# Late weight tiles and attention tiles at multiples of 64 bytes, and a start signal sent ahead of the first loads

## The chip, the cores and the metric

One Trainium2 chip, one NeuronCore of it. The metric is the device time of one execution in microseconds (us); lower is better. The engines are TensorE (PE; its weight loads are PEld), VectorE (DVE), ScalarE (ACT), GpSimd (POOL) and SyncE (SP), which issues most transfers.

## The reference

```python
# attention: q, k, v of (2, 8, 768, 64); proj of (64, 6)
q_bits = einsum('bhsd,dk->bhsk', q, proj) > 0          # 6 hash bits a row, the same for k
mask = q_bucket[:, :, :, None] == k_bucket[:, :, None, :]
scores = where(mask, q @ k.T / 8, -1e9)
attn = exp(scores - max); attn /= sum(attn) + 1e-9
x = (attn @ v).transpose(0, 2, 1, 3).reshape(1536, 512)
# layer 0: w_in (512, 2048), w_out (2048, 512)
h = x @ w_in
g = (a0 + a1*h + a2*h*h + a3*h**3) / (1 + |b0|*|h| + |b1|*h*h + 1e-6)
x = g @ w_out
# layer 1: the same sizes
h = x @ w_in
x = (h - tanh(h)) @ w_out
```

All of it is float32.

## The kernel before, in words

**Attention.** The 16 heads are worked in 8 pairs of two. A pair has 12 tiles of 128 queries by 768 keys. For each tile TensorE computes the scores (4 matmuls of 384 columns, L249), turns the tile before it with six transposes against `ident` (L375, from `E` into `turn_ps`) and, in 3 of 4 positions of a schedule, multiplies by v (4 matmuls of 384 columns, L333 and L335). VectorE takes the row minimum (L567), ScalarE the exponential (L455); the turned tile is split into a rounded part and a rest (`pt_hi` by ScalarE, `pt_lo` by VectorE). The operands of the scores are `qA`, `kA`, `qB`, `kB`, two sets of them for the two heads.

**The two layers.** All products are three matmuls of 512 columns, of rounded parts and rests (`_hi`, `_lo`). The 1536 tokens are 3 chunks of 512; the hidden 2048 are 16 tiles. That makes 48 tiles in each layer, 96 in all, numbered t. For tile t `pe_g1` makes h from x with 12 matmuls (L789, stationary operand `win`), and `pe_g2` multiplies g by `wout` with 12 matmuls (L818). In layer 0 `wout` is the stationary operand, in layer 1 it is the one that moves. TensorE's order is fixed: `pe_g1(t + 4)`, `pe_g2(t)`, `pe_g1(t + 5)`, and so on; the first four `pe_g1` stand between the last pieces of the attention. In layer 0 VectorE has seven operations of 512 columns for each tile; in the first chunk it also splits most weights, one `win_lo` and one `wout_lo` for a tile, since the weights of each layer are split when they are first used. `pe_g2(t)` waits for `g_lo(t)` of VectorE.

**Where tiles lie.** SBUF tiles are given out one behind the other. Each begins at a multiple of 32 bytes. The activations `x_hi`, `x_lo`, `g_hi`, `g_lo`, the early weights (`win0` to `win3`, `wout0`, `wout1`) begin at byte 16512 or a whole number of 128 bytes behind it. Behind the early weights stand five small tiles of 4 to 16 bytes, 32 bytes each. Their 160 bytes are two and a half times 64. So everything behind them begins at 32 bytes past a multiple of 64: the late weights (`win4` to `win15`, `wout2` to `wout15`, hi and lo), and the attention's `v_nat`, `bits`, `qA` to `kB` and `pats`. Then `counts`, 8 bytes in 32, brings `proj_bd`, `ident`, `E`, `v_hl`, `pt_hi` and `pt_lo` to a multiple of 64 (64 bytes past a multiple of 128); behind the small `row_` tiles `x_raw`, `x_pair`, `x_norm` and `scale` are at 32 past again. The late weights take the same space as the attention's tiles, once these are free.

**The start.** `pe_scores` of the first tile of a head waits for 128 counts of `ops0` or `ops1` for each pair done. From the second pair on these come from the eight copies of 16 counts that fill the operands. The first pair's operands are written by the engines themselves, so SyncE adds the 128 counts by hand (L1216, L1217). It does so behind all its starting loads, the six early weights among them.

Of the kernel before, what the change touches and what calls it, by code (L numbers as in the profile page):

```python
# [6 lines left out]
F32 = mybir.dt.float32  # L7
# [6 lines left out]
P = 128  # L14
# [16 lines left out]
def build(nc, q, k, v, proj, w_in1, w_out1, coef_a, coef_b, w_in2, w_out2,  # L31
          identity, patterns, bit_counts, out):
    B, H, S, D = q.shape
# [25 lines left out]
    top = ExitStack()  # L59
    att = ExitStack()  # L60
    mlp = ExitStack()
    sb = lambda ctx, name, shape, dt: ctx.enter_context(nc.sbuf_tensor(name, shape, dt))
# [11 lines left out]
            for names in ADDED_BY.values() for name in names}  # L74
    loads = {name: top.enter_context(nc.semaphore("s_" + name))
             for name in ["ident", "consts", "coefs", "ready", "coef", "proj", "q", "k", "v", "out", "ops0", "ops1",
                          "scale_out0", "scale_out1", "scale_in0", "scale_in1", "shift0", "shift1", "pool_here", "sync_here"]
             + ["t_turn", "t_q", "t_k", "t_dots", "t_bits", "t_hot", "t_hot_q", "t_hot_k",
                "t_hi_q", "t_hi_k", "t_hi_kb", "t_lo", "t_op1"]
             + [f"w_in{j}" for j in range(J)] + [f"w_out{j}" for j in range(J)]}  # L80
# [10 lines left out]
    with top:  # L91
# [37 lines left out]
        q_one = sb(top, "q_one", [P, 1], F32)  # L129
        sum_eps = sb(top, "sum_eps", [P, 1], F32)  # L130


        v_nat = sb(att, "v_nat", [P, 2, T * D], F32)
        bits = sb(att, "bits", [P, HALF], BF16)
# [1 line left out]
               for e in range(2)]  # L136
        opA, opB = [ops[e][0] for e in range(2)], [ops[e][1] for e in range(2)]
        pats = sb(att, "pats", [P, 4, P], BF16)
        counts = sb(att, "counts", [P, 2], F32)
        proj_bd = sb(att, "proj_bd", [P, 2, KB], F32)  # L140
        ident = sb(att, "ident", [P, P], F32)
        E = sb(att, "E", [P, RING, S], F32)
        v_hl = [sb(att, f"v_hl{e}", [P, T, 2, D], F32R) for e in range(2)]
        pt_hi = sb(att, "pt_hi", [P, 2, T, HALF], F32R)
        pt_lo = sb(att, "pt_lo", [P, 2, T, HALF], F32R)
        row_min = sb(att, "row_min", [P, RING], F32)
        row_sum = sb(att, "row_sum", [P, 2, T], F32)
        row_eps = sb(att, "row_eps", [P, 2, T], F32)
        row_inv = sb(att, "row_inv", [P, 2, T], F32)
        x_raw = [sb(att, f"x_raw{e}", [P, S], F32) for e in range(2)]  # L150
        x_pair = sb(att, "x_pair", [P, S], F32)
        x_norm = sb(att, "x_norm", [P, S], F32)
        scale = sb(att, "scale", [P, S], F32)
        slot = [ps(att, f"slot{i}", [P, 2, 512]) for i in range(2)]
        turn_ps = [ps(att, f"turn_ps{i}", [P, 512]) for i in range(2)]
        pv_ps = ps(att, "pv_ps", [P, 512])
# [332 lines left out]
        def dve_sum(eng, c):  # L489
            eng.wait_ge(mlp_sems["low"], c + 1)  # L490
            mine, _, cols = own_and_other(c)
            eng.tensor_tensor(x_raw[0][mine, cols], pv_ps[mine, 0:HALF], x_raw[0][mine, cols],
                              ALU.add).then_inc(mlp_sems["sum"], 1)
# [275 lines left out]
        def pe_g1(eng, t):  # L769
            layer, c, j = place(t)  # L770
            _, w_hi, w_lo = w_in_slot[j]
            if c == 0:
                if layer == 0 and j < POOL_IN:
                    eng.wait_ge(mlp_sems["early_lo"], POOL_TILES.index(("in", j)) + 1)
                else:
                    eng.wait_ge(mlp_sems["w_in_lo"], split_in_count(layer, j))
            if layer == 0 and c == 1 and j == 0:
                eng.wait_ge(sems["xlo"], BIAS + PAIRS - 1)
                eng.wait_ge(mlp_sems["last_lo"], 1)
            if layer == 1 and j == 0:  # L780
                eng.wait_ge(mlp_sems["x2_lo"], 4 * (c + 1))
            if t >= TILES_LAYER + 4:
                eng.wait_ge(mlp_sems["g"], t - 3)
            elif t >= 4:
                eng.wait_ge(mlp_sems["h_free"], t - 3)
            for kt in range(KT):
                ws = slice(kt * P, (kt + 1) * P)
                for n, (w, x) in enumerate(((w_lo, x_hi), (w_hi, x_hi), (w_hi, x_lo))):
                    mm = eng.matmul(h_ps[t % 4][:, :], w[:, ws], columns(x, kt, c),  # L789
                                    start=kt + n == 0, stop=kt == KT - 1 and n == 2)  # L790
            mm.then_inc(mlp_sems["h"], 1)

        def pe_g2(eng, t):
            layer, c, j = place(t)
            _, w_hi, w_lo = w_out_slot[j]
            hi, lo = g_hi[:, t % TEMPS, :], g_lo[:, t % TEMPS, :]
            if c == 0:
                if layer == 0 and j < POOL_OUT:
                    eng.wait_ge(mlp_sems["early_lo"], POOL_TILES.index(("out", j)) + 1)
                else:  # L800
                    eng.wait_ge(mlp_sems["w_out_lo"], split_out_count(layer, j))
            eng.wait_ge(mlp_sems["g_lo"], t + 1)
            if t == 0:
                eng.wait_ge(sems["pt_lo"], BIAS + 2 * TILES * PAIRS)
                eng.wait_ge(mlp_sems["sum"], GROUPS)
            for i in range(4):
                cs = slice(i * P, (i + 1) * P)
                if j == 0 and t > 0:
                    if layer == 0 or c == 0:
                        eng.wait_ge(mlp_sems["x2_raw"], 4 * (t // J - 1) + i + 1)  # L810
                    else:
                        eng.wait_ge(mlp_sems["y"], 4 * (c - 1) + i + 1)
                if layer == 0:
                    terms = ((w_lo[:, cs], hi), (w_hi[:, cs], hi), (w_hi[:, cs], lo))
                else:
                    terms = ((hi[:, cs], w_lo[:, :]), (hi[:, cs], w_hi[:, :]), (lo[:, cs], w_hi[:, :]))
                for n, (l, r) in enumerate(terms):
                    mm = eng.matmul(acc[i][:, :], l, r if layer else r[:, :], start=j + n == 0,  # L818
                                    stop=j == J - 1 and n == 2)
                if j == J - 1 and i < 3:  # L820
                    mm.then_inc(mlp_sems["acc"], 1)
            mm.then_inc(mlp_sems["g2"], 1)
# [253 lines left out]
        with nc.Block() as block:  # L1076

            @block.sync
            def _(eng):
# [86 lines left out]
                def load_weight(layer, kind, j):  # L1166
                    if kind == "in":
                        if layer == 1:
                            eng.wait_ge(mlp_sems["h"], 2 * J + j + 1)
                        w = (w_in1, w_in2)[layer]  # L1170
                        eng.dma_start(w_in_slot[j][0][:, :].rearrange("r (k n) -> r k n", n=P),  # L1171
                                      w.rearrange("(k r) n -> r k n", r=P)[:, :, j * P:(j + 1) * P]
                                      ).then_inc(loads[f"w_in{j}"], 16)
                    else:
                        if layer == 1:
                            eng.wait_ge(mlp_sems["g2"], 2 * J + j + 1)
                        w = (w_out1, w_out2)[layer]
                        eng.dma_start(w_out_slot[j][0][:, :], w[j * P:(j + 1) * P, :]
                                      ).then_inc(loads[f"w_out{j}"], 16)

                def sync_att(p, turn=True):
                    if turn:
                        load_qk(p + 2, 0)
                        load_qk(p + 2, 1)
                    copy_split(p + 1, 0)
                    if not is_zero(p):
                        shift(p - 1, 1)
                    scale_out(p, 0)
                    copy_hot(p + 1, 0)
                    load_v(p + 1)  # L1190
                    copy_split(p + 1, 1)
                    copy_hot(p + 1, 1)
                    scale_in(p, 0)
                    shift(p, 0)
                    scale_out(p, 1)
                    scale_in(p, 1)

                for e in range(2):
                    eng.dma_start(nat[0][:, :, e, :], q_d[0, :, e]).then_inc(loads["q"], 16)
                eng.wait_ge(loads["ready"], 1)  # L1200
                for x in range(2):
                    for e in range(2):
# [10 lines left out]
                    load_weight(0, "in", j)  # L1213
                for j in range(EARLY_OUT):
                    load_weight(0, "out", j)

                eng.sem_inc(loads["ops0"], 128)  # L1217
                eng.sem_inc(loads["ops1"], 128)
                sync_att(0)
                with eng.Fori(1, PAIRS - 2) as p:  # L1220
                    sync_att(p)
# [131 lines left out]
```

## Time and profile before

| | us |
|---|---|
| median of 3 runs | 783.09 (781.21 to 783.39) |
| the profiled execution | 782.13 |
| its span | 780.0 |
| TensorE busy | 766.5 (98%) |
| VectorE busy | 537.1 (69%) |
| ScalarE busy | 478.8 (61%) |
| GpSimd busy | 155.7 (20%) |

The span runs from the first to the last instruction that the profiler recorded; 2.13 us of the execution lie around it. In the timeline a row gives the start and the length of an instruction. The length of a matmul contains its latency: consecutive ones overlap, so TensorE's pace is read from the distance between starts.

### The profile page before, as it was taken

How to read it: one execution, taken by the hardware profiler on the slowest of the kernel's cores; microseconds unless marked ns; L12 is line 12 of the kernel's file. 1: busy time of each engine (PE TensorE's matmuls, PEld its weight loads, DVE VectorE, ACT ScalarE, POOL GpSimd, SP SyncE). 2: the span in 40 equal slices, each digit the busy share in tenths (PEclk: the TensorE clock that was granted, in tenths of full speed). 3: DMA queues.
4: the chain of work that ended last, by engine and by line, in shares of the span. 5: the costliest groups of instructions: out<-in, count | busy, mean ns of one | idle time of the engine just before them, and what ended most of it. 6: DMA issues, size and time to landing. Idle time of an engine off the chain costs nothing.

```text
span 780.0 us, 11965 instructions
## 1 busy us (share of the span) xinstructions
PE 766.5 (98%) x3840; PEld 645.0 (83%) x3840; DVE 537.1 (69%) x856; ACT 478.8 (61%) x940; POOL 155.7 (20%) x133
## 2 busy tenths in 40 slices
PE   4999999999999999999999999999999999999998
PEld 3899999999998877888888888888888888888886
DVE  3888988988997999999888888946442322232222
ACT  4888988988997878787666867755432222212221
POOL 5774575566566000000000000000000000000000
PEclk8999999999999999999999999999999999999999
DMA  7579778777744320000000232320000100001001
GB/s 192 122 171 208 171 174 190 184 177 175 170 116 122 119 82 1 1 0 1 1 0 15 56 106 84 106 67 1 1 0 1 55 0 1 1 14 41 0 1 55
DMA packets 65243, 58.11 MB, mean 75 GB/s; under 512 B 31792, under 2 KB 50480, under 8 KB 65200
## 3 DMA queue, kind: packets, MB, share of 16 engines
q1 hardware_dynamic: 63488, 57.09, 29.1%
q10 hardware_dynamic: 1712, 0.46, 0.3%
q8 instruction: 25, 0.41, 0.2%
q14 instruction: 18, 0.15, 0.1%
HBM read 29.57 MB, written 3.19 MB: 42 GB/s over the span
## 4 chain that ended last, share of the span: by engine, by line
PE 97%; DMA 1%; issue 1%; SPq 1%; ACT 0%; ACTq 0%; DVE 0%
PE acc L818 34%; PE h_ps L789 34%; PE slot L249 9%; PE turn_ps L375 8%; PE pv_ps L333 4%; PE pv_ps L335 4%; PE aux_ps L262 1%; PE aux_ps L271 1%; PE aux_ps L282 1%; DMA k_nat<-in_k 1%; SPq L1171 0%; PE turn_ps L292 0%; ACT E L455 0%; SPq L1091 0%; ACT kA L427 0%
## 5 line engine op out<-in xcount | busy, mean ns | idle before, releaser
L789 PE MATMUL h_ps<-x_hi,win_hi 128*128 128x512 f32 x384 | 152.1, 396 | 0.0
L789 PE MATMUL h_ps<-x_hi,win_lo 128*128 128x512 f32 x384 | 151.4, 394 | 0.0
L789 PE MATMUL h_ps<-x_lo,win_hi 128*128 128x512 f32 x384 | 150.9, 393 | 0.0
L839 ACT ACTIVATE g_hi<-pol 128x512 fp32r<-128x512 f32 x96 | 60.9, 634 | 128.2 <-PE acc L818 105.5
L1008 DVE TENSOR_TENSOR g_lo<-pol,g_hi 128x512 fp32r<-128x512 f32 x96 | 65.9, 686 | 102.1 <-ACT g_hi L839 101.9
L609 DVE TENSOR_TENSOR pt_lo<-turn_ps,pt_hi 128x384 fp32r<-128x384 f32 x192 | 97.9, 551 | 18.9 <-ACT pt_hi L516 17.2
L516 ACT ACTIVATE pt_hi<-turn_ps 128x384 fp32r<-128x384 f32 x192 | 84.2, 494 | 16.4 <-PE turn_ps L375 14.7
L567 DVE TENSOR_REDUCE row_min<-slot 128x1 f32<-128x768 f32 x96 | 90.5, 943 | 4.1 <-PE slot L249 4.1
L455 ACT ACTIVATE E<-slot,row_min 128x768 f32<-128x768 f32 x96 | 88.0, 917 | 5.4 <-DVE row_min L567 2.7
L789 PEld LDWEIGHTS h_ps<-x_hi,win_lo 128*128 128x128 f32 x384 | 72.1, 188 | 17.6
L789 PEld LDWEIGHTS h_ps<-x_lo,win_hi 128*128 128x128 f32 x384 | 72.1, 188 | 16.9
L789 PEld LDWEIGHTS h_ps<-x_hi,win_hi 128*128 128x128 f32 x384 | 72.1, 188 | 16.7
L1002 DVE TENSOR_TENSOR pol<-h_ps,mag 128x512 f32<-128x512 f32 x48 | 33.2, 691 | 70.7 <-ACT mag L862 70.7
L375 PE MATMUL turn_ps<-ident,E 128*128 128x128 f32 x576 | 80.2, 275 | 0.0
L862 ACT ACTIVATE mag<-h_ps 128x512 f32<-128x512 f32 x48 | 28.8, 600 | 81.4 <-PE h_ps L789 78.2
L818 PE MATMUL acc<-g_hi,wout_hi 128*128 128x512 f32 x192 | 76.4, 398 | 0.0
L818 PE MATMUL acc<-wout_hi,g_lo 128*128 128x512 f32 x192 | 75.9, 396 | 0.0
L818 PE MATMUL acc<-g_hi,wout_lo 128*128 128x512 f32 x192 | 75.9, 396 | 0.0
L818 PE MATMUL acc<-wout_lo,g_hi 128*128 128x512 f32 x192 | 75.9, 395 | 0.0
L818 PE MATMUL acc<-wout_hi,g_hi 128*128 128x512 f32 x192 | 75.9, 395 | 0.0
L818 PE MATMUL acc<-g_lo,wout_hi 128*128 128x512 f32 x192 | 75.3, 392 | 0.0
L375 PEld LDWEIGHTS turn_ps<-ident,E 128*128 128x128 f32 x576 | 68.4, 141 | 5.5 <-DVE pt_lo L609 1.7
(119 smaller groups left out, 1379.6 us busy)
## 6 DMA issues: line engine op xcount, KB each, us to landing
win_raw<-in_moe_w_in SPq DMA_DIRECT2D x32, 256.0 KB, 3.1
wout_raw<-in_moe_w_out SPq DMA_DIRECT2D x32, 256.0 KB, 2.8
q_nat<-in_q SPq DMA_DIRECT2D x16, 192.0 KB, 3.5
v_nat<-in_v SPq DMA_DIRECT2D x8, 384.0 KB, 3.5
scale<-softmax_scale SPq DMA_DIRECT2D x16, 192.0 KB, 3.2
k_nat<-in_k SPq DMA_DIRECT2D x14, 192.0 KB, 3.6
qA<-q_hi SPq DMA_DIRECT2D x14, 192.0 KB, 2.6
qB<-q_hi SPq DMA_DIRECT2D x14, 192.0 KB, 3.0
```

The costliest lines, as they stand in the source:

```text
L249: mm = eng.matmul(slot[m % 2][:, h, 0:HALF], ops[e][0][:, i * P:(i + 1) * P], ops[e][1][:, h * HALF:(h + 1) * HALF], start=first, stop=not ...
L333: eng.matmul(pv_ps[:, 0:HALF], vv, pt_hi[:, c % 2, kt, :], start=kt == 0, stop=False)
L375: mm = eng.transpose(turn_ps[h][:, c3 * P:(c3 + 1) * P], E[:, n % RING, kt * P:(kt + 1) * P], ident[:, :])
L455: eng.activation(halves(E[:, m % RING, :]), slot[m % 2][:, :, 0:HALF], ACT.Exp, bias=row_min[:, m % RING:m % RING + 1], scale=-1.0, accum_ ...
L516: eng.activation(pt_hi[:, c % 2, k0:k0 + T // 2, i * P:(i + 1) * P], turn_ps[h][:, 0:HALF].rearrange("r (k n) -> r k n", n=P), ACT.Copy).t ...
L567: eng.tensor_reduce(row_min[:, m % RING:m % RING + 1], slot[m % 2][:, :, 0:HALF], AX.XY, ALU.min).then_inc(sems["rowmin"], 1)
L609: eng.tensor_tensor(pt_lo[dst], turn_ps[h][:, 0:HALF].rearrange("r (k n) -> r k n", n=P), pt_hi[dst].bitcast(F32), ALU.subtract).then_inc( ...
L789: mm = eng.matmul(h_ps[t % 4][:, :], w[:, ws], columns(x, kt, c), start=kt + n == 0, stop=kt == KT - 1 and n == 2)
L818: mm = eng.matmul(acc[i][:, :], l, r if layer else r[:, :], start=j + n == 0, stop=j == J - 1 and n == 2)
L839: eng.activation(g_hi[:, t % TEMPS, :], pol[:, t % TEMPS, :], ACT.Copy).then_inc(mlp_sems["g_hi"], 1)
L1002: eng.tensor_tensor(pol[:, t % TEMPS, :], h_ps[t % 4][:, :], mag[:, t % 2, :], ALU.subtract).then_inc(mlp_sems["g"], 1)
L1008: eng.tensor_tensor(g_lo[:, b, :], pol[:, b, :], g_hi[:, b, :].bitcast(F32), ALU.subtract).then_inc(mlp_sems["g_lo"], 1)
```

## The change

Two things. A tile `filling` of 24 bytes (32 with the rounding) is put behind the five small ones, so that everything behind it begins 32 bytes later, at a multiple of 64. In the attention `counts` and the small `row_` tiles move behind all the large ones, so `ident`, `E`, `v_hl`, `pt_hi` and `pt_lo` stay where they were and `x_raw`, `x_pair`, `x_norm`, `scale` come to multiples of 64. The late weights then begin 64 bytes past a multiple of 128. No instruction is added or removed for it. The second: SyncE's two additions to `ops0` and `ops1` go from behind its starting loads to right behind the two loads of `q_nat`.

```diff
@@ -129,6 +129,8 @@
         sum_eps = sb(top, "sum_eps", [P, 1], F32)
 
+        sb(top, "filling", [P, 6], F32)
+
@@ -136,21 +138,21 @@
         pats = sb(att, "pats", [P, 4, P], BF16)
-        counts = sb(att, "counts", [P, 2], F32)
         proj_bd = sb(att, "proj_bd", [P, 2, KB], F32)
         ident = sb(att, "ident", [P, P], F32)
         E = sb(att, "E", [P, RING, S], F32)
         v_hl = [sb(att, f"v_hl{e}", [P, T, 2, D], F32R) for e in range(2)]
         pt_hi = sb(att, "pt_hi", [P, 2, T, HALF], F32R)
         pt_lo = sb(att, "pt_lo", [P, 2, T, HALF], F32R)
+        x_raw = [sb(att, f"x_raw{e}", [P, S], F32) for e in range(2)]
+        x_pair = sb(att, "x_pair", [P, S], F32)
+        x_norm = sb(att, "x_norm", [P, S], F32)
+        scale = sb(att, "scale", [P, S], F32)
         row_min = sb(att, "row_min", [P, RING], F32)
         row_sum = sb(att, "row_sum", [P, 2, T], F32)
         row_eps = sb(att, "row_eps", [P, 2, T], F32)
         row_inv = sb(att, "row_inv", [P, 2, T], F32)
-        x_raw = [sb(att, f"x_raw{e}", [P, S], F32) for e in range(2)]
-        x_pair = sb(att, "x_pair", [P, S], F32)
-        x_norm = sb(att, "x_norm", [P, S], F32)
-        scale = sb(att, "scale", [P, S], F32)
+        counts = sb(att, "counts", [P, 2], F32)
@@ -1197,6 +1199,9 @@
                 for e in range(2):
                     eng.dma_start(nat[0][:, :, e, :], q_d[0, :, e]).then_inc(loads["q"], 16)
+
+                eng.sem_inc(loads["ops0"], 128)
+                eng.sem_inc(loads["ops1"], 128)
                 eng.wait_ge(loads["ready"], 1)
@@ -1213,9 +1218,6 @@
                 for j in range(EARLY_OUT):
                     load_weight(0, "out", j)
-
-                eng.sem_inc(loads["ops0"], 128)
-                eng.sem_inc(loads["ops1"], 128)
                 sync_att(0)
```

SyncE at the start, before: these rows are its starting loads in their order. The additions are no rows of their own; they stand between the last row of `wout_raw` and the `q_nat` row that waits for `s_aux`, which is the first transfer of `sync_att(0)`.

```order
L1100 DMA v_nat<-in_v 128x2x384
L1091 DMA q_nat<-in_q 128x6x64 [waits s_t_turn]
L1091 DMA q_nat<-in_q 128x6x64
L1091 DMA k_nat<-in_k 128x6x64 [waits s_t_turn]
L1091 DMA k_nat<-in_k 128x6x64
L1210 DMA ca<-in_moe_a 128x4
L1211 DMA cb<-in_moe_b 128x2
L1171 DMA win_raw<-in_moe_w_in 128x4x128 x4
L1178 DMA wout_raw<-in_moe_w_out 128x512 x2
L1091 DMA q_nat<-in_q 128x6x64 [waits s_aux]
```

The same engine after the change: the additions stand between the first two rows here, ahead of all the others.

```order
L1201 DMA q_nat<-in_q 128x6x64 x2
L1208 DMA proj_bd<-in_proj 64x6 [waits s_ready]
L1208 DMA proj_bd<-in_proj 64x6 x3
L1210 DMA pats<-in_patterns 128x512
L1211 DMA counts<-in_bit_counts 128x2
L1102 DMA v_nat<-in_v 128x2x384
L1093 DMA q_nat<-in_q 128x6x64 [waits s_t_turn]
```

Of the loads themselves none changes its place; the additions have moved ahead of 16 transfers.

TensorE, before, at the first scores: `s_ops0` is one of seven semaphores that its first matmul of L249 waits for.

```order
L307 MATMUL aux_ps<-bits,pats 128x384 [waits s_t_bits,s_consts]
L307 MATMUL turn_ps<-bits,pats 128x384
L307 MATMUL pv_ps<-bits,pats 128x384
L307 MATMUL turn_ps<-bits,pats 128x384
L249 MATMUL slot<-kA,qA 128x384 [waits s_t_hot_q,s_t_lo,s_t_hot_k,s_t_hi_kb,s_ops0,s_t_hi_k,s_t_hi_q]
```

TensorE, after, at the same place.

```order
L309 MATMUL aux_ps<-bits,pats 128x384 [waits s_t_bits,s_consts]
L309 MATMUL turn_ps<-bits,pats 128x384
L309 MATMUL pv_ps<-bits,pats 128x384
L309 MATMUL turn_ps<-bits,pats 128x384
L251 MATMUL slot<-kA,qA 128x384 [waits s_t_hot_q,s_t_lo,s_t_hot_k,s_t_hi_kb,s_ops0,s_t_hi_k,s_t_hi_q]
```

Nothing has moved on TensorE but the line numbers, by two; only the time at which `s_ops0` is given changes.

## Rows read from the trace of the kernel before

**Rows 1.** The page: the chain that ended last, by engine.

```profile
PE 97%; DMA 1%; issue 1%; SPq 1%; ACT 0%; ACTq 0%; DVE 0%
```

**Rows 2.** Waits of TensorE: engine, line, releaser, us in total, times, longest.

```profile
PE slot L249 <- SPq L1217: 2.4, 1, 2.4
```

**Rows 3.** Timeline around the first scores: start us, us, engine, line, operation.

```profile
13.34 0.98 SPq L1178 DMA_DIRECT2D wout_raw<-in_moe_w_out  x2
...
14.52 0.59 PE L249 MATMUL slot<-kA,qA 128*128 128x384 f32 x2 [2.37 <-SPq L1217]
...
15.50 0.96 DVE L567 TENSOR_REDUCE row_min<-slot 128x1 f32<-128x768 f32 x1 [1.39 <-PE slot L249]
```

**Rows 4.** The chain, in order of time: start, us, what.

```profile
13.00 1.04 ACT kA L427 x2
```

**Rows 5.** Stretches: busy us (PE, PEld, DVE, ACT, POOL), granted clock, DMA.

```profile
12.20:14.50 2.30, 0.00 (x0) 0.01 (x1) 1.87 (x4) 1.82 (x4) 2.09 (x4) 1.00 0.90 258
...
15.50:22.00 6.50, 5.46 (x21) 4.88 (x20) 3.98 (x5) 3.76 (x9) 5.54 (x6) 0.50 0.34 114
```

**Rows 6.** Timeline of TensorE: the transposes of the first three tiles.

```profile
19.09 1.48 PE L375 MATMUL turn_ps<-ident,E 128*128 128x128 f32 x6
...
22.63 0.82 PE L375 MATMUL turn_ps<-ident,E 128*128 128x128 f32 x6
...
24.94 0.82 PE L375 MATMUL turn_ps<-ident,E 128*128 128x128 f32 x6
```

**Rows 7.** Timeline: `pe_g1(3)`, early weights, 12 matmuls up to 250.66.

```profile
248.17 0.39 PE L789 MATMUL h_ps<-x_hi,win_lo 128*128 128x512 f32 x1
...
250.66 0.40 PE L789 MATMUL h_ps<-x_lo,win_hi 128*128 128x512 f32 x1
```

**Rows 8.** Timeline: a late `win` in layer 0, 12 matmuls, then L818.

```profile
396.60 0.39 PE L789 MATMUL h_ps<-x_hi,win_lo 128*128 128x512 f32 x1
...
399.40 0.39 PE L818 MATMUL acc<-g_hi,wout_lo 128*128 128x512 f32 x1
```

**Rows 9.** Timeline, layer 1: the last nine matmuls of an early `win`, then L818.

```profile
592.89 0.39 PE L789 MATMUL h_ps<-x_hi,win_lo 128*128 128x512 f32 x1
...
594.93 0.40 PE L818 MATMUL acc<-wout_lo,g_hi 128*128 128x512 f32 x1
```

**Rows 10.** Timeline, layer 1: a late `wout` that moves, 12 matmuls, then L789.

```profile
600.48 0.40 PE L818 MATMUL acc<-wout_lo,g_hi 128*128 128x512 f32 x1
...
603.28 0.39 PE L789 MATMUL h_ps<-x_hi,win_lo 128*128 128x512 f32 x1
```

**Rows 11.** Timeline, layer 0: an early `win` between late tiles, 12 matmuls, then L818.

```profile
323.96 0.40 PE L789 MATMUL h_ps<-x_hi,win_lo 128*128 128x512 f32 x1
...
326.73 0.39 PE L818 MATMUL acc<-g_hi,wout_lo 128*128 128x512 f32 x1
```

**Rows 12.** Timeline: the last four of twelve L333, L335 ahead of 248.17 begin.

```profile
247.47 0.33 PE L333 MATMUL pv_ps<-pt_hi,v_hl 128*128 128x384 f32 x1
```

**Rows 13.** Timeline: scores and L333, L335 behind transposes; `pe_g1(0)` behind transposes.

```profile
232.26 0.60 PE L249 MATMUL slot<-kA,qA 128*128 128x384 f32 x2
...
233.75 0.82 PE L375 MATMUL turn_ps<-ident,E 128*128 128x128 f32 x6
234.33 0.48 PE L789 MATMUL h_ps<-x_hi,win_lo 128*128 128x512 f32 x1
...
236.25 0.39 PE L789 MATMUL h_ps<-x_lo,win_hi 128*128 128x512 f32 x1
```

**Rows 14.** A stretch of layer 0, columns as in the stretches above.

```profile
250.00:300.00 50.00, 50.00 (x215) 39.89 (x214) 49.84 (x78) 40.23 (x71) 0.00 (x0) 1.00 0.32 98
```

**Rows 15.** Timeline: `g_lo` and the first matmul of `pe_g2(10)`; the last matmul.

```profile
309.09 0.67 DVE L1008 TENSOR_TENSOR g_lo<-pol,g_hi 128x512 fp32r<-128x512 f32 x1
...
309.94 0.44 PE L818 MATMUL acc<-g_hi,wout_lo 128*128 128x512 f32 x1
...
776.39 0.40 PE L818 MATMUL acc<-wout_hi,g_lo 128*128 128x512 f32 x1
```

## The prediction, made before the change was run

> **What bounds the kernel now.** I read the chain that ended last first: 97% of it is TensorE, 0% VectorE and ScalarE [rows 1]. Then TensorE's waits: of those at the scores the largest is 2.4 us, once, for SyncE at L1217, the very signal that the change moves [rows 2]. Nothing behind the first scores is listed that is longer than 1 us. So the time is the sum of TensorE's starts, and the question for each part is whether it shortens a wait there, or the distance between two starts. The page cannot show the second: it gives every 512-column matmul some 395 ns, which contains latency. I therefore read the timeline for starts, tile by tile, and divided.
>
> **The signal.** SyncE's last load ahead of the signal is issued at 13.34 and takes 0.98, so it ends at 14.32; the scores start at 14.52, 0.20 later, after 2.37 us of idle [rows 3]. The first scores wait for six more signals. The last of those by the timeline is the second of ScalarE's four L427 operations: the third begins at 13.00 [rows 4], so the second is done by then. With the same 0.2 us for the signal the scores can begin at about 13.2, 1.3 us earlier. Does that carry on? VectorE's row minimum begins 0.98 us behind the scores [rows 3], so at about 14.2; VectorE is in its four L559 operations until about then (it has 1.87 us of work in the 2.30 before 14.5 [rows 5]), so it is just free. The copies for the next pair, GpSimd's splits and the loads hang on TensorE's own tiles and come earlier with them. Moving the signal puts two additions ahead of SyncE's loads; they are no transfers, and the addition after the loads took part of 0.20 us. If they delay the load of `proj` by 0.1 us, it is hidden or costs 0.1. I take **-1.3**. The bounds are 0, if something unseen holds the scores (or SyncE's later start), and -2.4, the whole wait.
>
> **The clock at the start.** In the 2.3 us before the scores TensorE did nothing, at a granted clock of 1.00 (2.4 GHz). From 15.5 to 22.0 the clock was 0.50 (1.2 GHz) [rows 5]. From the first tile's transposes to the second's it took 22.63 - 19.09 = 3.54 us, from the second's to the third's, at the full clock, 24.94 - 22.63 = 2.31 [rows 6]. The two stretches hold the same kinds of work, so the half clock cost 1.2 us there; for the scores between 15.5 and 19.09, which partly hide in waits for the exponential, I estimate 0.6 more. After the change the idle stretch is 1.3 us shorter. It may be that the clock then doesn't fall: -1.8. Or it falls over denser work: the 6.5 us at half clock hold 5.46 us of TensorE's work [rows 5], half of which, 2.7, would be lost if no gap hid any, where 1.8 is lost now: +0.9. I take **0** and keep both ends.
>
> **The late weights.** This is the main term. `pe_g1(3)` uses early weights, which are at multiples of 64 already, and follows matmuls on `v_hl` and `pt_hi`, which are too. From its first start, 248.17, to its twelfth, 250.66, are 11 gaps in 2.49 us: 226.4 ns each [rows 7]. A late `win` in the same layer takes 399.40 - 396.60 = 2.80 us for 12: 233.3 ns [rows 8]. In layer 1, where the other engines do little, the last nine gaps of an early `win` take 594.93 - 592.89 = 2.04: 226.7 ns [rows 9]. There the late `wout` is the operand that moves, and 12 take 603.28 - 600.48 = 2.80 again: 233.3 [rows 10]. So there are two paces, 226.6 and 233.3, and with the same clock, columns and type they go with the place of the weights. The traffic of the other engines doesn't explain them, since both paces are in both layers.
>
> One row seems to speak against it: an early `win` standing between late tiles takes 326.73 - 323.96 = 2.77 us, 230.8 ns [rows 11]. But in rows 9 the slow gaps are the first three of the twelve and the rest is fast, so I read this as a transient behind a slow group. With all groups alike it has no cause left. Another doubt is the early weights' place, a multiple of 128, where the late ones come to 64 past one. `v_hl` and `pt_hi` are 64 past one: the last four of a run on them take 248.17 - 247.47 = 0.70, 175 ns for 384 columns [rows 7, 12]; their pure columns' time is 0.75 of that at 512, so 226.6 would stand for about 170 to 173, 233.3 for 175 to 180. That is open, and leans to neither side by much; the twelve gaps of `pe_g1(3)` directly behind them at 226.4 without a transient say that they count as fast.
>
> The price: from the first start of `pe_g2(10)`, 309.94, to the last, 776.39 [rows 15], are 86 tiles of `pe_g2` and 81 of `pe_g1`, 2004 matmuls, so 2003 gaps in 466.45 us, 232.9 each. At 226.6 they take 453.9: **-12.6**.
>
> **Where it is not paid.** Before 309.94 it is otherwise. VectorE is busy 49.84 of the 50 us from 250 to 300 [rows 14], and `g_lo(10)` ends at 309.09 + 0.67 = 309.76, 0.18 before `pe_g2(10)` begins [rows 15]: TensorE has caught up with VectorE, which has its splits of the weights besides its seven operations. A faster TensorE waits here. Of the 250 to 310 stretch I take **0**; if all of it came too, its some 250 matmuls at 6.7 ns would give 1.7. Behind it VectorE's splits end and it runs ahead: `pe_g2` at 24 x 226.6 = 5.44 us a tile is still slower than seven operations of the 0.67 that `g_lo` takes, 4.7.
>
> **The attention.** `qA` to `kB` move to multiples of 64. Four scores and four products with v behind transposes take 233.75 - 232.26 = 1.49 us. `pe_g1(0)`, whose operands are all at multiples of 64, takes 236.25 - 234.33 = 1.92 for its first eight behind transposes [rows 13], 0.11 more than 8 x 226.6. If 384 columns at the fast pace are 226.6 less 128 columns at 2.4 GHz, 173.3, the scores' eight are 0.10 over 8 x 173.3. The start behind transposes costs the same with and without the alignment. I take **0**; the lower bound is the full 6.7 ns on 384 matmuls of the scores, -2.6. The copies and x tiles are off the chain (DMA 1% [rows 1]).
>
> **Sum.** 782.13 - 1.3 - 12.6 = 768.2. The median of the three runs is 0.96 above the profiled execution, so against it 769.2. I say **768.6**.
>
> **A rule against it.** The rows show two paces for tiles 32 bytes apart [rows 7, 8]. The Trainium skill, "SBUF — State Buffer", Specifications, says that a line of SBUF is 16 bytes and that crossing to new lines is what costs. 32 is a multiple of 16, so by that rule 32 bytes more change nothing for a matmul. The trace doesn't agree with it as the whole story, unless another property of the late weights makes the pace; the rival that this gives is the first below.
>
> **Rivals.**
> 1. *The place modulo 64 isn't it* (it is another property of the late tiles, or 128 counts): only the signal is left, 782.1 - 1.3 = 780.8. For it: all slow tiles are also the high ones, loaded late. Against it: `wout` and `win`, stationary and moving, are alike. 13%.
> 2. *Half of it*: the transients stay, and the pace is that of rows 11, 230.8: 2003 x 2.1 = 4.2, so 776.6. 7%.
> 3. *Slower*: 64 past a multiple of 128, against activations at multiples of 128, is a worse place than 32 past. If it costs over the present pace as much as that costs over the fast one, 6.7 ns, the 2003 gaps give +13.4 and the time is 794. It decides from 0.7 ns on, where it eats the 1.3. Against it stands `pe_g1(3)` behind `pt_hi`. 4%.
> 4. *Forecast*, 768.6, 76%; its own range, with the clock, the attention's bound and the stretch before 310, is 764 to 770.5.
>
> **Numbers.** 764 to 777 takes in the forecast and rival 2, some 82%. A measurement of this kernel tells 0.3%, 2.3 us, from no change. Faster: the forecast, rival 2 and a little of rival 1 if the clock stays up, 0.84. Same: the rest of rival 1, 0.12. Slower 0.04.
>
> **What would show it.** The wait for SyncE gone and the first scores at 13.2; the 12 matmuls of a late tile in 2.72 us in both layers, `pe_g2` every 5.44; gaps longer than 250 ns at `pe_g2` between tiles 4 and 10, with VectorE without idle; tile times of the attention unchanged at 2.3. The prediction is wrong if late tiles still take 2.80, or if VectorE holds `pe_g2` beyond tile 11.

## The result, and the profile after

The changed kernel takes 776.09 us (median of 4; 774.23 to 776.73), the kernel before 783.24 in the same measurement (median of 4; 781.21 to 783.39). The ratio is 0.9915, with a 95% interval of 0.9901 to 0.993: 7.15 us faster, a little under half of the 14.5 that lie between 783.09 and the forecast of 768.6. It is inside the range and close to the time of rival 2, whose mechanism is not what happened, as the experiments below show.

The profiled execution took 774.23 and its span 772.1, 7.9 less than the profiled one of before. The page has the same look: TensorE's busy time is 8 us less, the others' are hardly changed, and VectorE now holds 5% of the chain.

```profile
PE 758.5 (98%) x3840; PEld 642.3 (83%) x3840; DVE 537.0 (70%) x856; ACT 477.8 (62%) x940; POOL 155.4 (20%) x133
...
PE 91%; DVE 5%; issue 1%; ACT 1%; ACTq 0%; DVEq 0%
```

In TensorE's waits, the one for SyncE [rows 2] is gone. The wait for `kA` stands in its place, and a new one for `g_lo` is listed (columns as there).

```profile
PE slot L251 <- ACT E L457: 1.5, 1, 1.5
...
PE slot L251 <- ACT kA L429: 1.1, 1, 1.1
PE acc L820 <- DVE g_lo L1010: 0.6, 1, 0.6
```

The timeline of the first scores (start, length, what): the last early load is still issued at 13.29 [rows 3], but the scores no longer wait for it. They begin at 13.46 and wait for the second of ScalarE's four L429 operations, which is done when the third begins, at 13.16.

```profile
13.16 1.04 ACT L429 ACTIVATE kA<-turn_ps,counts 64x384 fp32r<-64x384 f32 x2
13.29 0.98 SPq L1180 DMA_DIRECT2D wout_raw<-in_moe_w_out  x2
13.46 0.59 PE L251 MATMUL slot<-kA,qA 128*128 128x384 f32 x2 [1.15 <-ACT kA L429]
14.44 0.96 DVE L569 TENSOR_REDUCE row_min<-slot 128x1 f32<-128x768 f32 x1 [0.17 <-PE slot L251]
```

The stretches of the start (us; busy PE, PEld, DVE, ACT, POOL; granted clock; DMA): from 15.5 to 22.0 the granted clock is 1.00 (2.4 GHz), where it was 0.50 (1.2 GHz) before [rows 5], with more work done by VectorE, ScalarE and GpSimd in that time.

```profile
12.00:13.40 1.40, 0.32 (x2) 0.00 (x0) 1.37 (x3) 1.28 (x3) 1.34 (x2) 1.00 0.94 205
15.50:22.00 6.50, 5.33 (x36) 4.52 (x37) 4.67 (x8) 6.03 (x15) 6.02 (x7) 1.00 0.41 128
```

The timeline of TensorE, that answers to [rows 6, 15]: the transposes of the first three tiles, then `pe_g2(10)` and the last matmul.

```profile
17.39 0.82 PE L377 MATMUL turn_ps<-ident,E 128*128 128x128 f32 x6
...
19.61 0.82 PE L377 MATMUL turn_ps<-ident,E 128*128 128x128 f32 x6
...
22.05 0.82 PE L377 MATMUL turn_ps<-ident,E 128*128 128x128 f32 x6
...
306.99 0.47 PE L820 MATMUL acc<-g_hi,wout_lo 128*128 128x512 f32 x1
...
768.53 0.39 PE L820 MATMUL acc<-wout_hi,g_lo 128*128 128x512 f32 x1
```

The 7.9 us can be laid out along these starts. First scores: 14.52 to 13.46, -1.06. From there to the third tile's transposes: 24.94 - 14.52 = 10.42 before, 22.05 - 13.46 = 8.59 now, -1.83. Then nothing changes up to `pe_g2(10)`; from one pair of heads to the next it is 28.01 us where it was 28.02, and from `pe_g2(0)` to `pe_g2(10)` 56.27 where it was 56.24. From `pe_g2(10)` to the last matmul: 466.45 before, 768.53 - 306.99 = 461.54 now, **-4.91** where -12.6 was forecast.

A late tile of layer 0 shows why it is less. Twelve matmuls from the first start to the next tile's take 2.75 us, 229 ns each; before it was 2.80 [rows 8].

```profile
342.90 0.39 PE L791 MATMUL h_ps<-x_hi,win_lo 128*128 128x512 f32 x1
...
345.65 0.39 PE L820 MATMUL acc<-g_hi,wout_lo 128*128 128x512 f32 x1
```

And where in layer 1 the late `wout` is the moving operand, nothing was gained at all: 618.36 - 615.55 = 2.81, as in [rows 10].

```profile
615.55 0.39 PE L820 MATMUL acc<-wout_lo,g_hi 128*128 128x512 f32 x1
...
618.36 0.40 PE L791 MATMUL h_ps<-x_hi,win_lo 128*128 128x512 f32 x1
```

### The profile page after: what moved, and what is told of

It is laid out like the page before. It is cut to its first block, busy times and chain, and to the rows that moved or that the text cites. A ratio compares the mean times of both kernels' runs of the same rounds, so it can differ in the third digit from the quotient of the medians.

```text
span 772.1 us, 11965 instructions
## 1 busy us (share of the span) xinstructions
PE 758.5 (98%) x3840; PEld 642.3 (83%) x3840; DVE 537.0 (70%) x856; ACT 477.8 (62%) x940; POOL 155.4 (20%) x133
## 4 chain that ended last, share of the span: by engine, by line
PE 91%; DVE 5%; issue 1%; ACT 1%; ACTq 0%; DVEq 0%
PE acc L820 32%; PE h_ps L791 31%; PE slot L251 9%; PE turn_ps L377 8%; PE pv_ps L335 4%; PE pv_ps L337 4%; PE aux_ps L264 1%; DVE sqr L965 1%; PE aux_ps L273 1%; PE aux_ps L284 1%; DVE pol L986 1%; DVE pol L972 1%; DVE pol L997 1%; DVE g_lo L1010 0%; DVE pol L978 0%
```

## The experiments

Eleven kernels. All compute the whole result. They ran in three measurements, each with the kernel before beside them: its medians were 782.36 (12 executions, E1 to E4), 782.45 (16, E5 to E8) and 782.63 (13, E9 to E11).

### E1 and E2: the two parts apart

E1 is the kernel before with the signal moved, E2 the changed kernel with the signal put back. The edit of E1 (that of E2 is its reverse):

```diff
@@ SyncE's start
                     eng.dma_start(nat[0][:, :, e, :], q_d[0, :, e]).then_inc(loads["q"], 16)
+
+                eng.sem_inc(loads["ops0"], 128)
+                eng.sem_inc(loads["ops1"], 128)
                 eng.wait_ge(loads["ready"], 1)
...
-                eng.sem_inc(loads["ops0"], 128)
-                eng.sem_inc(loads["ops1"], 128)
                 sync_att(0)
```

> The kernel before with SyncE's two additions moved ahead and every tile where it was. In the trace after the change the first scores begin 1.06 us earlier, and the granted clock does not fall at the start. If both are the signal's, this kernel gains 1.1 us from the signal and 1.8 to 2.0 from the clock: 779 to 780 against 782 to 783, with the first score matmul at 13.4 to 13.5 us, pe_g1(0) at 231.3 to 231.5, and the pace of late weights unchanged at 233.3 ns. The rival: the clock is chance from run to run, and only 1.1 us is the signal's: 781 to 782, with a stretch of half clock in the trace.

> The changed kernel with SyncE's two additions put back behind its starting loads: only the places of the tiles differ from the kernel before. Behind the start of pe_g2(10) the changed kernel takes 4.9 us less than before, 3.7 of it in layer 0 and 1.2 in layer 1, and between the first scores and pe_g1(0) 2.0 less. If those 2.0 are the clock's and the clock is the signal's, this kernel gains 4.9 and is at 777 to 778. If they come from the attention's tiles at multiples of 64, it gains 6.9 and is at 775 to 776.

E1: 780.2 (779.18 to 781.6, 6 executions), ratio 0.9972 (0.9959 to 0.9985), so -2.2. E2: 776.91 (776.05 to 778.32, 6), ratio 0.9933 (0.9919 to 0.9946), so -5.5. The two add up to 7.7, as much as the change within its uncertainty. The traces keep them apart too: from `pe_g2(10)` to the last matmul E1 takes 775.35 - 308.93 = 466.42 us, as the kernel before does (466.45), and E2 takes 771.65 - 310.08 = 461.57, as the changed kernel does (461.54). E2's rows:

```profile
310.08 0.47 PE L820 MATMUL acc<-g_hi,wout_lo 128*128 128x512 f32 x1
...
771.65 0.39 PE L820 MATMUL acc<-wout_hi,g_lo 128*128 128x512 f32 x1
```

E1's executions lie in two groups: 779.18, 779.27, 779.32 and 781.08, 781.1, 781.6, some 1.9 apart. The profiled one is of the slower group; its scores begin at 13.51, and its clock fell:

```profile
13.51 0.59 PE L249 MATMUL slot<-kA,qA 128*128 128x384 f32 x2 [1.15 <-ACT kA L427]
```

```profile
15.00:21.00 6.00, 5.07 (x19) 4.49 (x19) 3.58 (x5) 3.66 (x9) 5.52 (x6) 0.50 0.44 139
```

So the signal itself brings 1.0 us in the profiled execution, with the clock down in both kernels. The rest goes with the clock. Every execution has its mean granted clock on record: it is 1.000 in E1's three of 779.18 to 779.32 and 0.995 or 0.996 in its three of 781.08 to 781.6. The fall is worth what the changed kernel's profile shows between its first scores and its third tile, 1.8. E2's profiled execution (777.39, mean clock 0.996) has it too: its scores begin at 14.60 and its third tile's transposes at 25.23, 10.63 later where the kernel before took 10.42, so the attention's new places gained nothing there.

The moved signal is not what decides about the fall. The kernel before goes without it, or with a short one, as well: 18 of its 41 executions beside these experiments have a mean clock of 0.998 or more, down to 780.19 us, and 23 have 0.993 to 0.996. Whether the fall is rarer with the signal moved was not tested by itself.

A listed mean of 1.000 does not prove that there was no fall. The profiled execution of E6 (below) has 1.000 and is 2.9 slower than the fastest of its kernel; the stretch from 15.5 to 22.0 is listed at 1.00, but its first transposes take 1.48, and 3.37 to the next, as in the kernel before at 0.50 [rows 5, 6]. So its matmuls went at the pace of the lower level, and the listed clock does not show it. Its rows, and the stretch (columns as above):

```profile
13.65 0.98 PE L251 MATMUL slot<-kA,qA 128*128 128x384 f32 x2 [0.86 <-ACT kA L429]
...
18.90 1.48 PE L377 MATMUL turn_ps<-ident,E 128*128 128x128 f32 x6
...
22.27 0.82 PE L377 MATMUL turn_ps<-ident,E 128*128 128x128 f32 x6
```

```profile
15.50:22.00 6.50, 5.56 (x22) 4.95 (x21) 3.80 (x5) 3.95 (x9) 5.34 (x6) 1.00 0.32 110
```

Of the changed kernel's four, 774.23 is the profiled one (1.000, no fall), and 775.98 and 776.2 have 0.996, a fall. 776.73 has 1.000 and was not profiled; its cause is open.

### E3, E4, E5: every tile at one place

In the changed kernel the activations and early weights begin at multiples of 128, the late weights 64 past one. That leaves two explanations for the 2.75 and 2.81: the *place* (64 past 128 is worse than 0), or the *distance* between the two operands of a matmul. E3 puts the late tiles at multiples of 128 too. E4 puts everything, activations and early weights as well, 64 past a multiple of 128: the small tiles and the filling go ahead of `x_hi`. E5 is E4 without the filling: everything 32 past, the very place that was slow before. Distances between tiles are 0 modulo 256 in all three.

```diff
@@ E3
-        sb(top, "filling", [P, 6], F32)
+        sb(top, "filling", [P, 22], F32)
@@ E4 (E5: the same without the line of filling)
+        ca = sb(top, "ca", [P, 4], F32)
...
+        sum_eps = sb(top, "sum_eps", [P, 1], F32)
+
+        sb(top, "filling", [P, 6], F32)
         x_hi = sb(top, "x_hi", [P, KT, TOK], F32R)
...
-        ca = sb(top, "ca", [P, 4], F32)
...
-        sum_eps = sb(top, "sum_eps", [P, 1], F32)
-
-        sb(top, "filling", [P, 6], F32)
```

> The changed kernel with 64 bytes more of filling: late weights and attention tiles begin at multiples of 128, like the activations and the early weights. The trace after the change has three paces: 226.6 ns where both operands are at multiples of 128, 228.9 where the stationary one is 64 past, 233.3 where the moving one is 64 past. Theory A (each operand's own place modulo 128) and theory R (the distance between the two operands' places modulo 128) both say 226.6 for all tiles here: the 2003 gaps behind pe_g2(10) go from 461.8 to 453.9 us, so 7.9 less than the changed kernel's 774.2: 766 to 767. Theory H, in which what counts is the distance modulo a larger power of two (the late tiles stay 256 bytes off modulo 2048 from the early ones), says that the pace stays near that of the changed kernel: 772 to 775.

> The five small tiles and the filling stand ahead of the activations: all large tiles, activations, early and late weights and attention tiles, begin 64 past a multiple of 128, and at the same place modulo 2048 for weights and activations. Theory A (own place) says that every matmul now has a slow place, the early ones too: 233.3 ns throughout layer 1, 229 to 233 in layer 0, and 776 to 781. Theory R (distance) and theory H (distance modulo a larger power) say 226.6 everywhere: 766 to 767.

> The five small tiles stand ahead of the activations and there is no filling: every large tile begins 32 bytes past a multiple of 128, the place that the late weights had in the kernel before, but now the activations have it too. Theory R (distance) says 226.6 ns in both layers and 767 to 768 us. If 32 past is slow by itself, where 64 past is not, the pace is 233 ns and the time 780 or more.

E3: 767.33 (767.17 to 769.97, 5), ratio 0.9817 (0.9801 to 0.9833). E4: 767.33 (767.19 to 769.92, 5), 0.9825 (0.9809 to 0.9842). E5: 768.7 (767.25 to 770.25, 4), 0.9831 (0.9803 to 0.9859). The place by itself has no part in it, for the three that were tried, 0, 32 and 64 past a multiple of 128. Twelve matmuls take 2.72 us in all three. In E3, both layers:

```profile
359.57 0.39 PE L791 MATMUL h_ps<-x_hi,win_lo 128*128 128x512 f32 x1
...
362.29 0.39 PE L820 MATMUL acc<-g_hi,wout_lo 128*128 128x512 f32 x1
...
623.41 0.39 PE L820 MATMUL acc<-wout_lo,g_hi 128*128 128x512 f32 x1
...
626.13 0.39 PE L791 MATMUL h_ps<-x_hi,win_lo 128*128 128x512 f32 x1
```

In E5, where every operand is 32 past a multiple of 64:

```profile
623.95 0.39 PE L819 MATMUL acc<-wout_lo,g_hi 128*128 128x512 f32 x1
...
626.67 0.39 PE L790 MATMUL h_ps<-x_hi,win_lo 128*128 128x512 f32 x1
```

This is the pace of 226.6 ns that the prediction had counted on, and with it its time: 768.6 said, 767.3 to 768.7 measured.

### E6 and E7: other distances

The late tiles 128 off from the activations modulo 256 (E6), and at 96 modulo 256, 32 before the activations (E7). E6 asks if distances count modulo 128, E7 if a smaller one costs less.

```diff
@@ E6
-        sb(top, "filling", [P, 6], F32)
+        sb(top, "filling", [P, 54], F32)
@@ E7
-        sb(top, "filling", [P, 6], F32)
+        sb(top, "filling", [P, 14], F32)
```

> The changed kernel with 224 bytes of filling: late weights and attention tiles begin at multiples of 128, but 128 off from the activations modulo 256, where in the kernel with all tiles at 0 they were 0 off modulo 256. If the distance counts modulo 128, the pace is 226.6 ns again and the time 767 to 768. If it counts modulo 256 or more, there is a slower pace: at the 230 to 233 ns of the other distances, 772 to 780.

> The changed kernel with 64 bytes of filling: late weights 32 bytes short of the activations' place modulo 256, so the moving operand's place less the stationary one's is +32 in layer 0 and -32 for wout in layer 1, where it was +96 and -96 in the kernel before (233.3 and 233.3 ns) and +64 and -64 in the changed one (228.9 and 233.3). If the signed distance makes the pace, +32 should be no slower than +64: 226.6 to 229 in layer 0, and 227 to 233 in layer 1, 768 to 774 in all. If anything but 0 and 64 is as slow as before: 233 everywhere, 779 to 780.

E6: 778.98 (777.78 to 780.67, 8), ratio 0.9955 (0.9942 to 0.9968). E7: 778.7 (778.28 to 780.07, 9), 0.9957 (0.9946 to 0.9969). Both are slow: multiples of 128 for all tiles are not enough, and 32 bytes cost as much as 96. E6, twelve matmuls in 2.79 in layer 0 and 2.80 in layer 1:

```profile
362.75 0.40 PE L791 MATMUL h_ps<-x_hi,win_lo 128*128 128x512 f32 x1
...
365.54 0.39 PE L820 MATMUL acc<-g_hi,wout_lo 128*128 128x512 f32 x1
...
632.87 0.40 PE L820 MATMUL acc<-wout_lo,g_hi 128*128 128x512 f32 x1
...
635.67 0.40 PE L791 MATMUL h_ps<-x_hi,win_lo 128*128 128x512 f32 x1
```

### E8 and E9: has the distance a sign?

In the changed kernel a distance of 64 costs 2 ns where the activations move (layer 0; `pe_g1` of layer 1, which stands between slow groups, swings between 2.74 and 2.80) and 6.7 where the weight moves (`pe_g2` of layer 1). Either the distance has a sign (moving operand less stationary one: +64 there, -64 here), or it goes by which of the two moves, or by the layer. E8 starts from E3 and moves only `g_hi` and `g_lo` by 64: then `pe_g2` has +64 in layer 0 and -64 in layer 1, and `pe_g1` 0. E9 puts the late weights 64 on the other side of the activations, so that all signs of the changed kernel turn round.

```diff
@@ E8 (against E3)
         pol = sb(top, "pol", [P, TEMPS, CH], F32)
+        sb(top, "ahead_of_g", [P, 16], F32)
         g_hi = sb(top, "g_hi", [P, TEMPS, CH], F32R)
         g_lo = sb(top, "g_lo", [P, TEMPS, CH], F32R)
+        sb(top, "behind_g", [P, 48], F32)
@@ E9 (against the changed kernel)
-        sb(top, "filling", [P, 6], F32)
+        sb(top, "filling", [P, 38], F32)
```

> All tiles at multiples of 128 and 0 off modulo 256, but g_hi and g_lo 64 bytes further. g is the moving operand of pe_g2 in layer 0 and the stationary one in layer 1; pe_g1 doesn't touch it. Theory S (signed distance, moving less stationary: +64 gives 228.9 ns, -64 gives 233.3, as in the changed kernel) says 228.9 in layer 0's pe_g2 and 233.3 in layer 1's. Theory M (the role: an operand that moves from another place costs 233.3, a stationary one 228.9) says the opposite, 233.3 in layer 0 and 228.9 in layer 1. pe_g1 at 226.6 next to fast groups, up to 231 next to slow ones in both. Total 769 to 773 either way.

> The changed kernel with 160 bytes of filling: late weights 64 bytes on the other side of the activations' place modulo 256. Theory S (moving less stationary place modulo 256: 0 gives 226.6 ns, +64 gives 228.9, -64 gives 233.3) says that the changed kernel's paces change places: layer 0 and layer 1's pe_g1 now have -64, 233.3 ns, and layer 1's pe_g2, with the late wout moving, has +64 and 228.9. Total 777 to 779. If the sign doesn't matter, it is the changed kernel's 776.

E8: 775.27 (775.17 to 775.95, 4), ratio 0.9915 (0.9892 to 0.9938). E9: 779.66 (777.9 to 779.95, 5), 0.9956 (0.994 to 0.9971). In E8 `pe_g2` takes 2.76 in layer 0 and 2.80 in layer 1: by the role it would be the other way round, but it could still be the layer. E9 tells: in layer 0, where the changed kernel takes 2.75, it takes 2.80, and `pe_g2` of layer 1, 2.81 there, takes 2.77, at times 2.79, between two slow groups. The sign decides, not the role and not the layer. Its median is a little above the 777 to 779 expected; three of its five executions have the fall (0.996).

```profile
360.57 0.40 PE L791 MATMUL h_ps<-x_hi,win_lo 128*128 128x512 f32 x1
...
363.37 0.40 PE L820 MATMUL acc<-g_hi,wout_lo 128*128 128x512 f32 x1
...
630.91 0.40 PE L820 MATMUL acc<-wout_lo,g_hi 128*128 128x512 f32 x1
...
633.68 0.39 PE L791 MATMUL h_ps<-x_hi,win_lo 128*128 128x512 f32 x1
```

E8 also shows that the distance within a matmul is not all. Its time is above the 769 to 773 expected, since `pe_g1`, whose two operands are at distance 0, does not run at 2.72: it takes 2.77 in layer 0 and 2.75 in layer 1 between the `pe_g2` groups. E8's starts, two groups of layer 0 and `pe_g2` of layer 1:

```profile
359.58 0.40 PE L793 MATMUL h_ps<-x_hi,win_lo 128*128 128x512 f32 x1
...
362.35 0.40 PE L822 MATMUL acc<-g_hi,wout_lo 128*128 128x512 f32 x1
...
365.11 0.40 PE L793 MATMUL h_ps<-x_hi,win_lo 128*128 128x512 f32 x1
...
628.21 0.40 PE L822 MATMUL acc<-wout_lo,g_hi 128*128 128x512 f32 x1
...
631.01 0.39 PE L793 MATMUL h_ps<-x_hi,win_lo 128*128 128x512 f32 x1
```

The paces of the late tiles together. The distance is the place of the moving operand less that of the stationary one, modulo 256; the time of 12 matmuls is from starts as above; the last column is the distance of the first matmuls of `pe_g2` 16 tiles apart, 384 matmuls, from the same timelines. Of their 32 groups six are on early weights, at distance 0 but for `g` in E8.

| kernel | distance, layer 0 / layer 1 `wout` | 12 matmuls, us | 16 tiles, us |
|---|---|---|---|
| before | +96 / -96 | 2.80 / 2.80 | 89.40 / 89.36 |
| changed | +64 / -64 | 2.75 / 2.81 | 87.73 / 88.97 |
| E3, E4, E5 | 0 / 0 | 2.72 / 2.72 | 87.04 / 87.04 |
| E6 | 128 / 128 | 2.79 / 2.80 | 89.10 / 89.13 |
| E7 | +32 / -32 | 2.80 / 2.80 | 89.12 / 89.23 |
| E8 (`pe_g2`; `pe_g1` is at 0) | +64 / -64 | 2.76 / 2.80 | 88.53 / 88.75 |
| E9 | -64 / +64 | 2.80 / 2.77 | 89.28 / 89.02 |

### E10: does it matter in the attention?

The attention was at distance 0 before the change already: `q` and `k` were both 32 past a multiple of 64, and tiles of 3072 bytes are whole multiples of 256. So its term of 0 was no test. E10 takes E3 and sets `k` 96 from `q`, and `pt` 96 from `v_hl`.

```diff
+        def operand(n, part, e):
+            t = sb(att, f"{n}{part}{e}", [P, S], F32R)
+            sb(att, f"behind_{n}{part}{e}", [P, 24 if n == "q" else 40], F32)
+            return t
+        ops = [[[operand(n, part, e) for n in "qk"] for part in "AB"] for e in range(2)]
...
+        sb(att, "ahead_of_pt", [P, 24], F32)
         pt_hi = sb(att, "pt_hi", [P, 2, T, HALF], F32R)
```

> The kernel with all tiles at 0 (767.3), with kA, kB put 96 bytes on from qA, qB modulo 256, and pt_hi, pt_lo 96 on from v_hl; the layers are untouched. The attention's tiles had distance 0 in every kernel so far but by chance of sizes, and a pair took 28.01 us in all of them. Theory 1: that is why the change gained nothing in the attention, and with +96 each of the 768 matmuls of 384 columns costs up to 6.7 ns more, so a pair takes up to 0.6 us longer (28.3 to 28.6) and the whole 769 to 772. Theory 2: behind transposes the place of the operands doesn't matter; a pair stays at 28.01 and the whole at 767.3.

768.8 (767.91 to 771.51, 4), ratio 0.9834 (0.9811 to 0.9858). From a pair's second transposes to the next pair's it takes 28.06 us, against 28.01 in E3:

```profile
74.52 0.82 PE L381 MATMUL turn_ps<-ident,E 128*128 128x128 f32 x6
...
102.58 0.82 PE L381 MATMUL turn_ps<-ident,E 128*128 128x128 f32 x6
```

One pair takes 28.24. From the first scores to `pe_g1(0)` it is 218.53 us against 217.81 in E4, 0.7 us over the whole attention. The last twelve products with v, back to back, take 2.12 us where they take 2.11 in E3. In the attention's runs of 384 columns the distance costs next to nothing.

### E11: VectorE's bound before `pe_g2(10)`

The faster TensorE waits for VectorE there: in E3 a listed 0.73 us at `pe_g2(6)`, then 5.65 us a tile where 5.44 is TensorE's pace. E11 gives GpSimd the splits of 13 more late tiles, of which ScalarE did the rounded part and VectorE the rest.

```diff
@@ against E3
-                      + LATE[:FREE_SCORES])
+                      + LATE[:FREE_PV])
```

> The kernel with all tiles at 0, and GpSimd, idle from 250 us on, splits the first 20 late weights of layer 0 instead of 7; ScalarE and VectorE split only the last 6. If VectorE's splits are why TensorE waits 1.1 us ahead of pe_g2(6) and then runs at 5.65 us a tile to pe_g2(10), those waits go, 1.1 + 5 x 0.21 us, and perhaps the 0.6 at pe_g2(16): 764.5 to 765.3. If GpSimd's reads hold up VectorE, or its splits come too late, the time is 767 or more.

779.28 (778.21 to 781.43, 9), ratio 0.9964 (0.9951 to 0.9977): 12 us slower than E3. VectorE has fewer operations and yet is later: those with both inputs in SBUF take 1.5 to 2.4 times as long, those that read PSUM no longer than before. Groups of VectorE's instructions by shape, 252 to 282 us (last columns: busy us, mean ns, idle before), first E3, then E11:

```profile
L986 DVE SCALAR_TENSOR_TENSOR pol<-pol,ca,mag 128x512 f32<-128x512 f32 x5 | 3.7, 749 | 0.0
...
L978 DVE SCALAR_TENSOR_TENSOR pol<-pol,ca,h_ps 128x512 f32<-128x512 f32 x5 | 3.7, 744 | 0.0
```

```profile
L986 DVE SCALAR_TENSOR_TENSOR pol<-pol,ca,mag 128x512 f32<-128x512 f32 x4 | 7.3, 1816 | 0.0
...
L978 DVE SCALAR_TENSOR_TENSOR pol<-pol,ca,h_ps 128x512 f32<-128x512 f32 x4 | 2.9, 734 | 0.0
```

L986 takes two inputs from SBUF and goes from 749 to 1816 ns; L978, one of whose inputs is `h_ps` in PSUM, is unchanged. The Trainium skill, "SBUF — State Buffer", Who interferes with whom, says that a VectorE instruction with two SBUF inputs contends with a GpSimd instruction that reads SBUF; by that rule the trace agrees. TensorE then waits for `g_lo` four times, 8.8 us in all, and behind such a wait the granted clock fell to 0.50 as well, over work with no gap:

```profile
PE acc L820 <- DVE g_lo L1010: 8.8, 4, 4.2
```

```profile
281.00:285.00 4.00, 0.09 (x1) 0.00 (x0) 4.00 (x4) 2.06 (x4) 2.36 (x1) 1.00 0.00 0
286.00:289.00 3.00, 3.00 (x8) 2.30 (x7) 2.97 (x6) 2.20 (x4) 0.00 (x0) 0.50 0.03 5
```

## Why the prediction was right and wrong

**The signal: right.** The scores came forward by 1.06 us, 1.3 was said. They now hang on ScalarE's work on `kA`, as predicted; the third of its operations began at 13.16 instead of 13.00 [rows 4], which is 0.16 of the 0.26 missing. The two additions ahead of the loads cost nothing that shows. They have moved ahead of 19 transfers, by the rows of SyncE's loads, not 16; no sum uses the number.

**The clock at the start: the sum's 0 holds for one part of the executions.** The prediction had -1.8 as the lower end, and the profiled execution shows it, -1.83. That this execution, and not the one profiled of the kernel before, went without the fall is luck: E1 has three executions of each kind, and the kernel before has both kinds too. In the median of E1 this and the signal together are 2.2, 0.9 more than the term of 1.3.

**The late weights: the step that failed.** It was the sentence that, with the same clock, columns and type, the two paces "go with the place of the weights". They go with the distance between the places of the two operands modulo 256. The rows of before held both readings: the late tiles were 32 past a multiple of 64, and they were also 96 from the activations. Rows 13 hinted at it: the scores, whose `q` and `k` were both 32 past, stood as close to the fast pace (0.10 over) as `pe_g1(0)` (0.11 over), though they were at the place that was called slow. But they could not decide it, since the attention hardly shows a distance either: with 96 between the operands the same eight matmuls take 231.50 - 230.00 = 1.50 in E10, where they took 1.49. So no row of before told the place from the distance, and the distance had no rival of its own; it is one reading of the "another property" of rival 1, at 13%. The change left 64 between weights and activations, which is worth 4 ns of the 6.7 with one sign and nothing with the other: -4.91 from `pe_g2(10)` on, 3.66 of it in layer 0 and the rest in layer 1. The doubt that the prediction named and left open, 64 past a multiple of 128 against activations at multiples of 128, was the place where the 7.7 us went. As a prize for the fast pace everywhere, 12.6 was well sized: E3, at 767.33, is 15 below the kernel before, of which E1's part is 2.2, and from `pe_g2(10)` on the trace of E3 takes 761.90 - 307.30 = 454.60 us, 11.85 less than before.

**The transient.** That an early `win` at 2.77 between late tiles [rows 11] is a transient of a slow group was right: in E3 to E5, with all groups alike, there is none left behind `pe_g1(3)`. Where groups differ they come back: `pe_g2` of layer 1 in E9 takes 2.77 for 2.75, and `pe_g1` in E8 2.77 for 2.72.

**Where it is not paid: right.** From `pe_g2(0)` to `pe_g2(10)` TensorE stays bound by VectorE, 56.27 us for 56.24. The gap was among the tiles where it was expected, at the start of `pe_g2(6)`: 284.38 - 283.39 = 0.99 us.

```profile
283.39 0.39 PE L791 MATMUL h_ps<-x_lo,win_hi 128*128 128x512 f32 x1
284.38 0.47 PE L820 MATMUL acc<-g_hi,wout_lo 128*128 128x512 f32 x1 [0.60 <-DVE g_lo L1010]
```

**The attention: right, for another reason.** A pair took 28.01 for 28.02. Its tiles were at distance 0 before and after, and E10 shows that it would hardly have mattered.

**The rivals.** Rival 1 (only the signal, 780.8) was wrong in its time and right in its core: the place modulo 64 isn't it, as E5 shows. The rule that stood for it, lines of 16 bytes in "SBUF — State Buffer", Specifications, of the Trainium skill, isn't the whole story: 32, 64 and 96 are multiples of 16, and E7, the changed kernel and E3 differ only by such distances and by 11 us. Rival 2 had the time (776.6) with transients as its mechanism; the changed kernel's settled pace in layer 0 is 229 and needs none. Rival 3 fell: layer 1's `wout` is at 2.81, no worse than before.

**What stays open.** The trace doesn't say which accesses meet: a matmul's moving stream with its own stationary operand, or with the load of the next weights, which runs beside it. Nor why +64 and -64 differ, why a group at distance 0 is slowed by its neighbours (E8), or where between 0 and 32 the cost sets in. The runs show paces only, for 512 columns of this type.

## What to carry to other kernels

When TensorE is the bound, read the pace of identical matmuls from their starts and compare groups that differ only in which tiles they use; if there are two paces, tabulate both operands' places and look at their difference modulo 256 before their places. Giving every operand of the products the same place modulo 256 (sizes that are multiples of 256, small tiles in one block ahead or filled up to 256) cost one number in one line of the changed kernel here (E3) and took 15 us of 782 together with the signal. Before calling a property the cause, ask what else differs between the same rows, as the distance did here beside the place, and which kernel would change only one of the two, as E5 does. And don't take VectorE's work to GpSimd while VectorE is on the path with operands in SBUF.

## What the hardware showed that I had not expected

- A matmul of 512 columns at the full clock starts every 226.7 ns where all groups are at distance 0, 228.9 at +64, some 233 at 128, and 233.3 at -64, ±32 and ±96; the absolute place (0, 32 or 64 past a multiple of 128) makes no difference. A group at distance 0 between groups at +64 takes 2.77 us for 12 (E8), 231 ns.
- In the same kernel the clock at the start falls in some executions and not in others, for 1.9 us of the whole (E1: 779.18 to 779.32 at a mean of 1.000, 781.08 to 781.6 at 0.995 or 0.996). A listed 1.00 can hide it, as in E6's profile. E3 and E4 have slower executions too, 769.8 to 770.0 against 767.2 to 767.3, all at a listed 1.000; none of the slower ones was profiled, so their cause is open.
- An operation of VectorE with both inputs in SBUF went from 749 to 1816 ns beside GpSimd's splits.
